# Two of the sixteen first-half matmuls of an expert layer as 64-row matmuls in opposite halves of the array

## What is computed

```python
rms = np.sqrt(np.mean(x * x, axis=-1, keepdims=True) + 1e-06)
xn = x / rms * rms_g
g = xn @ w_gate                              # 1536 x 320 by 320 x 1536
silu = g * (1.0 / (1.0 + np.exp(-g)))
val = xn @ w_val
return (silu * val @ w_out).astype(np.float32)
```

## Time and profile before

| | us |
|---|---|
| runs | 563.83, 568.30, 569.98 (median 568.3) |
| span of the profiled execution | 565.6 |
| second layer, first matmul to last | 349.6 to 561.2 |

### The profile page before, as it was taken

The page is one execution under the profiler, slowest core; times in us unless marked ns, Lnnn a source line. Parts: engine busy times, 40 slices in busy tenths (PEclk is TensorE's granted clock), DMA queues, the critical chain, the costliest instruction groups (busy, mean ns, idle before and its releaser), DMA issues.

```text
span 565.6 us, 7912 instructions
## 1 busy us (share of the span) xinstructions
PE 495.2 (88%) x2582; PEld 428.4 (76%) x2582; DVE 368.5 (65%) x657; ACT 311.3 (55%) x595; POOL 235.9 (42%) x229
## 2 busy tenths in 40 slices
PE   1689888698599998978998798969999999999996
PEld 1479777497378887767877587858888888888886
DVE  6255687657699999899998999383434434353333
ACT  3935655432699998967989698643321212212121
POOL 6045565322388877756786766523420000000000
PEclk9985989769999999989999999979999999999999
DMA  6444656323000000000001100321200100010001
GB/s 227 126 125 125 195 160 199 101 70 93 1 13 22 14 13 13 12 13 12 13 28 29 28 2 0 85 55 35 80 1 1 46 1 1 0 48 0 1 0 48
DMA packets 29408, 28.79 MB, mean 51 GB/s; under 512 B 14424, under 2 KB 23000, under 8 KB 29368
## 3 DMA queue, kind: packets, MB, share of 16 engines
q1 hardware_dynamic: 29368, 28.29, 16.9%
HBM read 26.32 MB, written 1.97 MB: 50 GB/s over the span
## 4 chain that ended last, share of the span: by engine, by line
PE 48%; DVE 24%; issue 12%; ACT 6%; DMA 5%; POOL 2%; SPq 1%; DVEq 0%; ACTq 0%; POOLq 0%
DVE g L821 7%; PE ps L1073 6%; PE ps L1071 6%; PE ps L1072 6%; DVE nr L810 5%; DMA q_pair<-q_p_dram 5%; DVE nr L815 5%; PE ps L1039 4%; PE ps L1041 4%; PE ps L1040 4%; PE ps L949 4%; PE ps L976 4%; PE ps L1075 3%; PE ps L1076 3%; PE ps L985 2%
## 5 line engine op out<-in xcount | busy, mean ns | idle before, releaser
L1039 PE MATMUL ps<-wo_hi,g_hi 128*128 128x320 f32 x336 | 105.8, 315 | 4.8 <-DVE x_lo L852 2.9
L1041 PE MATMUL ps<-wo_hi,g_lo 128*128 128x320 f32 x336 | 104.9, 312 | 0.0
L1040 PE MATMUL ps<-wo_lo,g_hi 128*128 128x320 f32 x336 | 104.8, 312 | 0.0
L649 ACT ACTIVATE cc<-ps 128x512 f32<-128x512 f32 x36 | 21.5, 597 | 139.9 <-PE ps L1076 139.9
L435 POOL TENSOR_TENSOR qq<-qq,ab 128x512 f32<-128x512 f32 x48 | 63.2, 1318 | 56.7 <-ACT qq L577 53.8
L881 DVE TENSOR_TENSOR pp<-ps,cc 128x512 f32<-128x512 f32 x36 | 24.9, 691 | 92.9 <-ACT cc L649 92.9
L1039 PEld LDWEIGHTS ps<-wo_hi,g_hi 128*128 128x128 f32 x336 | 64.0, 191 | 9.1 <-DVE x_lo L852 3.3
L1040 PEld LDWEIGHTS ps<-wo_lo,g_hi 128*128 128x128 f32 x336 | 64.1, 191 | 2.9
L1041 PEld LDWEIGHTS ps<-wo_hi,g_lo 128*128 128x128 f32 x336 | 64.0, 191 | 0.0
L442 POOL TENSOR_TENSOR g_lo<-g,g_hi 128x512 fp32r<-128x512 f32 x48 | 62.7, 1307 | 1.8 <-ACT g_hi L597 1.5
L1024 PE MATMUL ps<-x_hi,w_hi 128*128 128x512 f32 x96 | 39.9, 415 | 14.6 <-DVE pp L802 14.6
(11 more groups left out here) (149 smaller groups left out, 1127.2 us busy)
## 6 DMA issues: line engine op xcount, KB each, us to landing
stage<-w_in_dram SPq DMA_DIRECT2D x20, 384.0 KB, 3.4
stage<-w_out_dram SPq DMA_DIRECT2D x8, 320.0 KB, 4.6
k_pair<-k_p_dram SPq DMA_DIRECT2D x12, 208.0 KB
q_pair<-q_p_dram SPq DMA_DIRECT2D x12, 208.0 KB
kn<-k_n_dram SPq DMA_DIRECT2D x12, 208.0 KB, 3.8
q_diag<-q_t_dram SPq DMA_DIRECT2D x24, 80.0 KB
v<-v_n_dram SPq DMA_DIRECT2D x12, 160.0 KB, 4.6
sig_o<-o_n_dram SPq DMA_DIRECT2D x2, 960.0 KB, 8.5
```

Source lines behind the costliest of these rows:

```text
L1039: pe.matmul(acc[t], hi, hi_w[:, f, :], start=(f == 0), stop=False)
L1040: pe.matmul(acc[t], hi, lo_w[:, f, :], start=False, stop=False)
L1041: mm = pe.matmul(acc[t], lo, hi_w[:, f, :], start=False, stop=(f == FT - 1))
```

## The change

For the stacked rest of the second layer, gate and value get opposite halves. Gate (first 128 columns of the stack) keeps high on partitions 0 to 63 and low on 64 to 127; value (last 128 columns) has low on 0 to 63 and high on 64 to 127. GpSimd's one subtract on 64 partitions and 256 columns becomes two on 64 partitions and 128 columns each. The product of the high rest with low x is then made with 64 rows only: for gate with partitions 0 to 63, for value with 64 to 127. These two matmuls come first in the unit and open the two banks (`start=True`); the other seven of each bank follow and add to them. The product low by low is no longer made. A unit has sixteen matmuls before and after.

```diff
-                own(pool.tensor_tensor(st[REM:P, part, :], src[REM:P, :, w:], st[REM:P, part, :].bitcast(F32), ALU.subtract))
+                if kind == "in1":
+                    own(pool.tensor_tensor(st[REM:P, part, :], src[REM:P, :, w:], st[REM:P, part, :].bitcast(F32),
+                                           ALU.subtract))
+                else:
+
+                    own(pool.tensor_tensor(st[REM:P, part, 0:P], src[REM:P, :, w:w + P],
+                                           st[REM:P, part, 0:P].bitcast(F32), ALU.subtract))
+                    own(pool.tensor_tensor(st[0:REM, part, P:], src[0:REM, :, w + P:],
+                                           st[0:REM, part, P:].bitcast(F32), ALU.subtract))
...
                 for m, bank in enumerate((gp[n % 2], vp[n % 2])):
+                    half = slice(m * REM, (m + 1) * REM)
+                    pe.matmul(bank, wst[half, at_, m * P:(m + 1) * P], x_lo[half, 2, cols], start=True, stop=False)
+                for m, bank in enumerate((gp[n % 2], vp[n % 2])):
                     for k in range(2):
                         c0 = (2 * m + k) * P
                         hi, lo = whi[:, at_, c0:c0 + P], wlo[:, at_, c0:c0 + P]
-                        pe.matmul(bank, hi, x_hi[:, k, cols], start=(k == 0), stop=False)
+                        pe.matmul(bank, hi, x_hi[:, k, cols], start=False, stop=False)
                         pe.matmul(bank, hi, x_lo[:, k, cols], start=False, stop=False)
                         pe.matmul(bank, lo, x_hi[:, k, cols], start=False, stop=False)
-                    st = wst[:, at_, m * P:(m + 1) * P]
-                    pe.matmul(bank, st, x_hi[:, 2, cols], start=False, stop=False)
-                    pe.matmul(bank, st, x_lo[:, 2, cols], start=False, stop=True).then_inc(in2_done, 1)
+                    pe.matmul(bank, wst[:, at_, m * P:(m + 1) * P], x_hi[:, 2, cols], start=False, stop=True)\
+                        .then_inc(in2_done, 1)
```

## The result

| | before | after |
|---|---|---|
| median of 20 runs, us | 564.49 (553.62 to 577.0) | 566.94 (560.67 to 574.1) |
| ratio, 95% interval | | 1.0083 [1.0044, 1.0122] |
| span of the profiled execution, us | 565.6 | 564.6 |

The change makes the kernel slower by 0.8%, 4.7 us (2.5 to 6.9). The ratio leaves out the slow runs, those over 1.5% above the fastest of the same kernel; the medians over all twenty are 2.45 us apart. The two profiled executions alone would say the opposite, and this is the first thing to read: their spans differ by -1.0 us, because the attention and the first expert layer, which the change leaves alone but for one GpSimd instruction, happened to take 6 us less in the one after. The first expert layer's first matmul starts at 136.9 us instead of 140.7, the second layer's first at 343.6 instead of 349.6. Cut at that matmul, the windows view of the kernel before gives

The account below looks back on a forecast made before the run. TensorE's own time was taken as the bound. Per unit -0.465 + 0.40 + 0.34 = +0.28 us, times 34 is +9.5, plus 0.2 for GpSimd, +9.7 on the 568.3 median: 578.0 us, range 560 to 582.

Parts of the forecast that it names:

- rival A: 64-row pair: no drain and the pair overlaps, gain 7.9 us to 560.4, or 4.1 us to 564.2; chance 0.27.
- the forecast's own 571.4 to 580.1: Time range in us for drains both ways with a side-by-side pair, given chance 0.50.
- drain case: Second-layer unit with array drains at both height changes: +0.28 us per unit, bounds +0.09 to +0.34.
- The bound and the units that count: Second layer: only TensorE's own time counts, and 34 of the 36 units lie on the path.
- The switch: Array height change, twice per unit: emptying plus exposed weight load, 0.16 to 0.23 us, taken as 0.20 each.
- The pair itself: Two 64-row matmuls per unit: 0.23 to 0.34 us, taken as 0.34 because the second starts 0.11 us later.
- the nearest row: Trace rows of successive weight loads, 0.11 us each at full clock, used to take the 64-row pair at 0.34 us.
- GpSimd, a term with the wrong sign: Split subtract: hidden in steady units, but 0.2 us (0 to 0.7) added where it runs beside VectorE's scaling at 370.97.
- The clock, a term put at nothing: Half-clock stretch from 377.2 to 380.2 us: worth up to 1.5 us either way, no change taken.
- B: Array height change: one direction needs no emptying, -0.03 to +0.08 us per unit, 567 to 571 us; chance 0.10.
- C: The two 64-row matmuls run one after the other: 568.5 without drain (chance 0.05), 582.1 with drains (chance 0.08).

Follow-up runs that it names:

- experiment 7: Changed kernel with only gate's low-x matmul at 64 rows and value's following at full height; unit 5.867 us, 0.226 more than the changed kernel.
- Experiment 6: Changed kernel with, from unit 12, two units' 64-row pairs run together, earlier units full height; 5.446 us per unit, 1.0008 [0.9948, 1.0067] against the kernel before.
- experiment 1: Changed kernel with both low-x matmuls back at full height, new order and split subtract kept; unit 5.481 us, 0.9962 [0.9855, 1.0069] against the kernel before.
- experiment 2: Changed kernel with the old stack, GpSimd's one subtract, and both 64-row matmuls on the same upper half; unit 5.875 us, 0.23 more.

## Why the prediction was off

The direction, and the mechanism with it, were right: TensorE is the bound, the height change drains the array both ways, and this outweighs the step saved. The size was twice too large: 9.7 us against 4.7 in the runs. By the prediction's own yardstick (1%, 5.7 us, to tell slower from same) the outcome belongs to "same", which it gave 0.32. That 566.9 lies between 560 and 582 says little, as that range was made to hold rival A at 560.4 too; of the forecast's own 571.4 to 580.1 it is outside. The measured change of a unit, 0.16 us, lies within the bounds of its drain case, 0.09 to 0.34.

- *The bound and the units that count:* held in the main. 34 x 0.160 = 5.4 us against 5.0 in the trace of the second layer and 4.7 in the runs. The 32 steady units make the 5.0; what units 0 to 3 lost, 0.5 us, came back before unit 4 (see GpSimd).
- *The switch, 0.20 us each, 0.40 per unit:* measured 0.386 (experiment 7). The sum of an emptying that lay between half and all of the slow row's 0.14 us and the exposed load of 0.09 was sound. Experiment 6 reads the parts of the switch back apart: 0.10 for the emptying, where 0.11 was taken, and 0.10 for the exposed load, where 0.09 was.
- *The pair itself, the step that failed.* The text said that the two weight loads come one after the other, and took 0.34 us "by the nearest row". It measured one step, 0.23 (in experiment 7 the second member and its load cost nothing): the loads into opposite halves go side by side as the matmuls do. The nearest row was of loads for the whole array, or for the same 16 rows; it bears on loads into the same rows of the array and not on these. My inference from it, that fewer rows don't make a load shorter, was true and beside the point: a load isn't shorter, there are two at once. This is 0.11 of the 0.12 us per unit by which the forecast was too high, 3.7 us of 9.7. With 0.23 the sum would have been 34 x 0.165 + 0.2 = 5.8 us. The Trainium skill, "TensorE: Matmul & The Clock Gate", Part 3, has matmuls in different row tiles start about 4 ns apart, and the pair here agrees to within the 0.01 us of its rows; the prediction had put that rule with the rival that has no drain, while it holds beside the drain.
- *GpSimd, a term with the wrong sign:* 0.46 + 0.45 us with 0.08 between them at 365 us, 1.0 in all as taken, and hidden in the steady units (experiment 1). The 0.2 us added for the collision with VectorE came out as 1.1 us saved. The prediction had read the earlier trace rows wrongly: the scaling of 1.57 us ran beside L408, the subtract of the full blocks, and the one beside the subtract L407 was the 64-column scaling of 0.81 us. With two short subtracts VectorE's last two scalings are over in 1.34 us instead of 2.42, and experiments 1 and 2 tie this to the split: in all seven traces with it the two last 0.54 to 0.56 and 0.76 us, in the two without it 0.81 to 0.83 and 1.57.
- *The clock, a term put at nothing:* it took most of this back. The stretch at half clock starts 23.8 us after the layer's first matmul before and 24.5 after and lasts 6.8 us in both traces, and the output matmuls now start 0.9 us earlier, so that more of them lie inside it: they take 5.81 us instead of 4.96. The prediction had allowed up to 1.5 us either way for this and taken none. So from the layer's first matmul to unit 4 are 32.52 us, before 32.57: units 0 to 3 cost 0.52 us, the transposes' stretch gives back 1.41, the scalings' 1.1 among it, the clock takes 0.85. In experiment 1, with the split and without the pair, it is 384.42 - 351.96 = 32.46 us, so the split by itself gained 0.1 us there.
- *The rest of the distance* lies in the base: 578.0 was put on a median of three runs, 568.3, and twenty give 564.5. This is 3.8 of the 11.1 us between 578.0 and 566.9.
- *Rivals:* A falls with the gaps marked "issue". B falls because neither direction is free: on the way in the pair starts 0.09 us later than a step of 0.147 would have it and the next step is 0.10 us too long (experiment 6), on the way out the emptying is 0.10 and the long step 0.11 too long. That 566.9 lies next to B's 567 to 571 comes from the lower base; its unit, -0.03 to +0.08 us, was not met. C falls with experiment 2.

## What to carry to other kernels

Packing two 64-row matmuls into opposite halves of the array does halve their time, but on a stream of full-height matmuls each excursion costs two drains with an exposed weight load, 0.39 us here, or 1.7 steps of 512 columns; by these prices it must replace at least four such matmuls at once to gain, and two units in one excursion (experiment 6) only just did, by 0.035 us per unit in the trace. Price a mode change by experiment 7's recipe: change one matmul of the stream and take the difference of the period. Where runs spread by per cents, measure the period of the loop in the trace and cut the span at the first instruction that the change touches. And where an engine off the path slows one that is on it, look at how long its single instructions are: splitting GpSimd's subtract freed VectorE 1.1 us earlier. Then check at what clock the work behind it now runs, as here it took most of this back.

## What the runs showed of the hardware

- Within 64-row mode there is no second drain: in experiment 6 the second pair follows the first after 0.33 us, as a full-height matmul follows the first one after a switch (0.34), and the end of the merged four is (0.73 - 0.49) = 0.24 us later than that of two, one step. The drain comes with the change of height alone.
- The one switch of the trace before, at the slow rate, took 0.30 us; at full clock one takes 0.19, the mean of the two directions. It neither halves nor stays.
- VectorE's scaling ends only after the GpSimd subtract beside it: 0.81 us beside one of 0.72, 0.55 beside one of 0.46, where the same scaling takes 0.28 with GpSimd idle. Why the scaling is held was not tested.
